# Score products of levels 2 to 6 by head, each head on its own half of TensorE's rows

## The reference

```python
def _attn_ref(q, k, v, f_logit):            # (4, 8, 768, 48)
    f = 1.0 / (1.0 + np.exp(-f_logit))
    state = np.zeros((B, H, D, D))
    for t in range(S):
        state = f[:, :, t, :, None] * state + np.einsum('bhd,bhe->bhde', k[:, :, t], v[:, :, t])
        y[:, :, t] = np.einsum('bhd,bhde->bhe', q[:, :, t], state)

def _moe_ref(x, w_in, w_out):               # (3072, 384) x (384, 2048) x (2048, 384)
    h = x @ w_in
    return (h * (1.0 / (1.0 + np.exp(-1.702 * h)))) @ w_out

def _moe2_ref(x, domain_probs, w1, w2):     # 4 experts, 384 -> 1024 -> 384
    p = domain_probs / (domain_probs.sum(-1, keepdims=True) + 1e-09)
    for e in range(E):
        out += p[:, e:e + 1] * (np.maximum(x @ w1[e], 0.0) @ w2[e])
```

## Time and profile before

| | |
|---|---|
| time, median of 3 runs | 1414.91 us (1414.72 to 1416.94) |
| profiled execution | 1414.12 us, of it the span 1412.4 us |
| granted clock of TensorE | 0.999 of full speed |
| PE busy | 1386.7 us, 98% of the span |
| DVE, POOL, ACT busy | 913.5, 629.6, 568.4 us |
| line 1580 | 960 pairs: 120 from half 0, 840 from halves 1 to 7 |
| share of line 1580 in the chain that ended last | 7% |

### The profile page before, as it was taken

How to read it: one execution, slowest core, us unless ns; L and a number is a source line. 1 busy time by engine, 2 the same in 40 slices (tenths; PEclk the granted TensorE clock), 3 DMA queues, 4 the chain that set the end, 5 groups by cost and what they waited for, 6 DMA issues and landing times.

```text
span 1412.4 us, 20981 instructions
## 1 busy us (share of the span) xinstructions
PE 1386.7 (98%) x8092; PEld 1311.8 (93%) x8092; DVE 913.5 (65%) x1376; ACT 568.4 (40%) x975; POOL 629.6 (45%) x719
## 2 busy tenths in 40 slices
PE   6899999999999999999999999999999999999999
PEld 5799999999999999999999999999999999999998
DVE  7785747566665656356566666666666666666666
ACT  5563534344444445245333233332333333433331
POOL 8686645556564747265512122211212454344430
PEclk9999999999999999999999999999999999999999
DMA  9535243332425160121011010101011112222111
GB/s 156 121 84 83 60 60 79 47 92 36 103 26 113 16 114 13 41 90 51 23 34 35 12 34 23 34 12 34 12 34 56 35 34 67 91 68 67 46 57 45
DMA packets 239796, 79.00 MB, mean 56 GB/s; under 512 B 188752, under 2 KB 238160, under 8 KB 239696
## 3 DMA queue, kind: packets, MB, share of 16 engines
q1 hardware_dynamic: 239696, 77.66, 23.9%
HBM read 67.83 MB, written 9.78 MB: 55 GB/s over the span
## 4 chain that ended last, share of the span: by engine, by line
PE 94%; POOL 2%; issue 1%; DVE 1%; ACT 1%; SPq 1%; DMA 0%; POOLq 0%; DVEq 0%; ACTq 0%
PE bank L1766 9%; PE bank L1764 9%; PE bank L1765 9%; PE bank L1700 9%; PE bank L1701 9%; PE bank L1699 9%; PE bank L1580 7%; PE bank L1672 5%; PE bank L1673 5%; PE bank L1674 5%; PE bank L1506 4%; PE bank L1508 4%; PE bank L1507 4%; PE bank L1612 3%; PE bank L1620 1%; PE bank L1629 1%
## 5 line engine op out<-in xcount | busy, mean ns | idle before, releaser
L1460 DVE SCALAR_TENSOR_TENSOR acc<-bank,p_n,acc 128x384 f32<-128x384 f32 x384 | 235.0, 612 | 68.0 <-PE bank L1766 62.9
L788 POOL TENSOR_TENSOR g_l<-sig,g_h 128x384 fp32r<-128x384 f32 x128 | 163.8, 1280 | 228.6 <-ACT g_h L1027 228.6
L1766 PE MATMUL bank<-w_h,h_l 128*128 128x384 f32 x768 | 257.3, 335 | 0.0
L1764 PE MATMUL bank<-w_h,h_h 128*128 128x384 f32 x768 | 257.2, 335 | 0.0
L1765 PE MATMUL bank<-w_l,h_h 128*128 128x384 f32 x768 | 257.0, 335 | 0.0
L1444 DVE TENSOR_TENSOR bank<-bank,x_copy 128x512 f32<-128x512 f32 x192 | 124.5, 694 | 166.0 <-ACT x_copy L1124 102.4
L1701 PE MATMUL bank<-xs,we_l 128*128 128x512 f32 x528 | 206.5, 391 | 0.0
L1700 PE MATMUL bank<-xs,we_h 128*128 128x512 f32 x528 | 206.4, 391 | 0.0
L1699 PE MATMUL bank<-xs,we_h 128*128 128x512 f32 x528 | 205.5, 389 | 0.7 <-issue 0.7
L839 POOL TENSOR_TENSOR we_l<-we_raw,we_h 128x384 fp32r<-128x384 f32 x96 | 97.2, 1037 | 213.4 <-ACT we_h L1092 213.4
L1356 DVE TENSOR_TENSOR sig<-bank,sig 128x384 f32<-128x384 f32 x128 | 71.0, 555 | 162.8 <-ACT sig L1020 161.4
(11 more groups left out here) (145 smaller groups left out, 2567.1 us busy)
## 6 DMA issues: line engine op xcount, KB each, us to landing
we_raw<-in_moe_w SPq DMA_DIRECT2D x32, 384.0 KB, 4.0
w_raw<-in_moe_w SPq DMA_DIRECT2D x32, 384.0 KB, 3.3
v_sb<-in_v SPq DMA_DIRECT2D x24, 192.0 KB, 3.5
x_dram<-work SPq DMA_DIRECT2D x8, 576.0 KB, 3.1
x_raw<-x_dram SPq DMA_DIRECT2D x12, 384.0 KB, 4.0
f_raw<-in_f_logit SPq DMA_DIRECT2D x56, 72.0 KB, 2.1
q_raw<-in_q SPq DMA_DIRECT2D x56, 72.0 KB, 2.1
k_raw<-in_k SPq DMA_DIRECT2D x56, 72.0 KB, 2.0
```

Source lines behind the costliest of these rows:

```text
L788: pool.tensor_tensor(g_l[:, j % RING, :], sig[:, j % 2, :], g_h[:, j % RING, :].bitcast(F32), ALU.subtract).then_inc(gl_ready, 1)
L1460: dve.scalar_tensor_tensor(acc[:, pr * TT + i, :], y_bank[y % 3][:, 0:DM], p_n[:, col:col + 1], acc[:, pr * TT + i, :], ALU.mult, ALU.add) ...
L1764: pe.matmul(dst, hh, wh, start=f == 0, stop=False)
L1766: last = pe.matmul(dst, hl, wh, start=False, stop=f == 1)
```

## The change

From half 1 on, `level_by_heads` takes the place of the loop over chunks. Each score product is done per head: weights are the head's 48 rows of `k_T`, 128 columns of them, and the streamed operand is the head's 64 columns of `q_split`. `tile_position=(0, 0)` for even and `(64, 0)` for odd heads places them on the upper or the lower 64 rows of the array. A level has 24 products of 64 columns instead of 12 of 128, so 48 recorded pairs instead of 24. For level 6 only the first 64 key positions are loaded (`rows`), since only they are wanted.

The banks no longer hold one chunk each. The bank `odd` holds the odd heads of chunks 0 and 1, `even` their even heads, and `last` both heads of chunk 2 in turn; upper and lower rows never write the same bank at a time, and before the odd heads of chunk 2 go into `last` TensorE waits for `upper_ready`. The readers get at their scores through `scores_of`, with as many elements as before. `unit_ready` is raised after products 16, 23 and 24 of the level's 24; before, it was raised after 4, 8 and 12 of 12. The level waits at its start for the banks `last` and `odd` and after eight products for `even`; before, each chunk waited for its own.

```diff
+    def scores_of(i, n):
+        if n == 0 or i == CH - 1:
+            return scores_T[:, i, :, :]
+        by_two = scores_T[:, 0:2, :, :].rearrange("p c (r j) x -> p (c r) j x", j=2)
+        return by_two[:, :, 1 - i, :]
...
-                    done = act.activation(scores_T[lo:lo + m, i, :, lo + m:lo + 2 * m],
+                    done = act.activation(scores_of(i, n)[lo:lo + m, :, lo + m:lo + 2 * m],
...
-                        dst = scores_T[:, i, :, :].rearrange("p h (b a m) -> p h b a m", a=2, m=m)[:, :, :, 1, :]
+                        dst = scores_of(i, n).rearrange("p h (b a m) -> p h b a m", a=2, m=m)[:, :, :, 1, :]
...
+            def level_by_heads(L, n):
+                odd, even, last = (level_unit[L] + i for i in range(CH))
+                def head(u, at, ch, r, j):
+                    x, lo = r * CH + ch, GAP * j
+                    rows = HALF_CH if L == LEVELS - 1 else P
+                    return pe.matmul(ring[u % 3][0:rows, at * HALF_CH:(at + 1) * HALF_CH],
+                                     k_T[lo:lo + D, x * P:x * P + rows], q_split[lo:lo + D, x, j, :],
+                                     start=True, stop=True, tile_position=(lo, 0))
+                bank_free(last, n)
+                bank_free(odd, n)
+                pe.wait_ge(split_ready, (n * (LEVELS - FIRST) + L - FIRST + 1) * 2 * CH)
+                pe.wait_ge(kg_ready, (n * LEVELS + L) * CH)
+                for r in range(PAIRS):
+                    upper = head(last, 2 * r, 2, r, 0)
+                    if r == PAIRS - 1:
+                        upper.then_inc(upper_ready, 1)
+                    head(odd, r, 0, r, 1)
+                bank_free(even, n)
+                for r in range(PAIRS):
+                    head(even, r, 0, r, 0)
+                    lower = head(odd, PAIRS + r, 1, r, 1)
+                lower.then_inc(unit_ready, 1)
+                for r in range(PAIRS):
+                    upper = head(even, PAIRS + r, 1, r, 0)
+                    if r == PAIRS - 1:
+                        upper.then_inc(unit_ready, 1)
+                    if r == 0:
+                        pe.wait_ge(upper_ready, (n - 1) * (LEVELS - FIRST) + L - FIRST + 1)
+                    lower = head(last, 2 * r + 1, 2, r, 1)
+                lower.then_inc(unit_ready, 1)
...
-                    if L < FIRST and not fine(n):
+                    if not fine(n):
+                        if L >= FIRST:
+                            level_by_heads(L, n)
                         return
```

More of the change, by code:

```diff
@@ L383, in moe_of_attention_kernel @@
         w_hi_ready, w_lo = sem("w_hi_ready"), {"pool": sem("w_lo_by_pool"), "dve": sem("w_lo_by_dve")}
-        unit_ready = sem("unit_ready")
+        unit_ready, upper_ready = sem("unit_ready"), sem("upper_ready")
         read_by = {"act": sem("act_read"), "dve": sem("dve_read")}
@@ L1569, in step @@
                         bank_free(u, n)
[L1570 to L1577, removed]
+                        pe.wait_ge(split_ready, (L - FIRST) * 2 * CH + 2 * (ch + 1))
+                        pe.wait_ge(kg_ready, (L - 1) * CH + ch + 1)
                         for r in range(PAIRS):
```

## The result

The changed kernel takes 1422.13 us (median of four runs, 1420.99 to 1423.69) against 1414.82 (1413.97 to 1416.94): 7.3 us slower, ratio 1.005 with an interval of 1.0033 to 1.0068. It is inside the forecast range of 1405 to 1502, on the slow side, and 4.6 us above the predicted 1417.5. The profiled execution took 1420.99 us, its span is 1419.3.

A forecast was written before the change was run, and what follows sets the result against it. TensorE was taken to bound the kernel. Terms 0 - 9.4 + 6.0 + 3.9 + 2.1 = +2.6 us on the profiled 1414.1 gave 1416.7, and 0.8 for the median made 1417.5 us; range 1405 to 1502.

The forecast's parts named there:

- the case: Loads of upper and lower rows run side by side: 1417.5 us, from 1405 to 1434, chance 48%.
- its signs: Profile after: levels 2 to 5 at 2.8 to 3.0 us, level 6 at 1.6 to 1.8, TensorE idle before level 6.
- loads in series: Rival: the array takes one weight load at a time, +81 us, 1496 us, chance 33%.
- (c): Entering and leaving a level changes the array's shape: 0.17 us a level, +6.0 us, range 0 to +12.
- (b): Level 6 loads only 64 weight columns, so it takes half the time: -1.34 us a level, -9.4 us.
- (d): At each level the lower half starts and ends one step later: 0.11 us a level, +3.9 us, or 0.
- (a): Levels 2 to 5: doubled loads run side by side in both halves, 0 us; one after the other, +75 us.
- (e): Later `unit_ready` delays ScalarE's squares at level 5, so TensorE waits 0.3 us before level 6: +2.1 us.
- Each half twice as quick: Rival: shorter loads make a level 1.34 us, -35 us in all, 1380 us, chance 13%.

The follow-up runs named there:

- level 6 alone: Only level 6 goes by heads, all other levels as in the kernel before: 1414.02 us against 1416.69, ratio 0.998.
- the kernel with the bands late: Kernel before with level 6 by heads and GpSimd's last small cross products and VectorE's sum moved behind tile 7's low part: 1436.86 us, ratio 1.0146.
- the second attempt's control: Kernel before, whole height, with GpSimd's low part of tile 7 ahead of its level 6 fade and k_rows transposes one slot later: 1419.82 us, ratio 1.0045.

## Why the prediction was right, and where it was off

The sum was +2.6 us and the outcome +7.3; the case was the forecast one, and its signs came: 2.83 and 1.61 us for the levels in the chain, 0.27 us at an entry, and an idle time ahead of level 6. That the time fell into the range says little by itself, since the range had to hold the loads in series too. That the sum is off by no more than 4.7 us is in part luck: (c), the gain of (b) and the missed wait were too favourable by 3.9, 1.2 and 1.1 us, (d) was too dear by 2.2.

**(a), loads side by side: right.** 48 pairs in the time of 24, and 4.90 us when each half's products stand together. This was the 75 us of the question, and the trace of before could not decide it; the argument that nothing shown as shared is asked for twice held, and the condition that it named, consecutive products on opposite halves, turned out to be needed. The Trainium skill (TensorEngine Tiling (Array Packing), Key Properties) says that different tiles load and multiply in parallel; the trace agrees where the halves alternate, 0.059 us a pair.

**(b), level 6: right, slightly too large.** 1.40 us from first to last matmul instead of 2.57, -1.17 a level where -1.34 stood: the step in each half is 0.059, not 0.056, and the first pair of the level is slower. -8.2 instead of -9.4 us.

**(c), the changes of shape: the mis-sized term.** I put 0.17 us a level, half of the 0 to 0.34 from the rows. The entry costs 0.10 and the exit 0.20, 0.30 together at levels 2 to 5 and 0.24 at level 6: +9.9 instead of +6.0 us, near the upper end. The same section of that page says that a change of the tiling mode drains TensorE. The trace agrees: the next load isn't started early, and each edge costs time. By that rule I had +8.6 us for the sum, and that is nearer to the 7.3 than my own value. The reason not to trust it, that no row of before showed such a change, was a reason for a wide range and none for the middle.

**(d), the second half starts a step late: wrong mechanism.** At levels 2 to 5 both halves start and end together, 0.007 us apart. A level is 0.06 us longer from its first to its last start, at its first pair, not 0.11: +1.7 us instead of +3.9.

**(e), the wait for ScalarE: right in place and size**, 0.31 us a half for 0.3 predicted, +2.2 for +2.1, and shown by level 5 whole against by heads. The size is in part luck: the squares start 0.91 us later in the level and not 0.7, but level 5 itself lasts longer, which gives ScalarE most of the difference back. Missed: GpSimd. I wrote that the time of its unit stays, which holds for the time within a level. But in the kernel before the low part of tile 7 was ready less than 0.1 us ahead of its use in `layer_out` (258.10 and 258.16), at the end of a chain over VectorE and GpSimd, and anything that delays these relative to TensorE, or makes TensorE earlier, ends in a wait there. In the changed kernel that is 0.16 us a half, +1.1; with level 6 alone it took 4.7 of 6.5 us.

The rivals: loads in series did not come, and would have with the same products in another order. Each half twice as quick is refuted at levels 2 to 5, where a half's step is 0.112 as ever; it is the load that bounds, and it goes by columns (0.112, 0.085 and 0.059 us a step at 128, 96 and 64) and not by rows. The chance of 61% for slower was right.

## What to carry to other kernels

Before two products are placed side by side, ask which of load and streaming sets the step: halving the streamed columns gains nothing while each product needs as many weight columns as before, and the gain comes only where both shrink. Count the edges: an excursion into another shape of the array costs 0.24 to 0.34 us here, so it needs at least that much work saved inside. Put products that are to overlap next to each other in the program: TensorE looked only some three pairs ahead. And a gain on the bounding engine stops at the next engine's margin: look for work that arrives within 0.1 us of its use, and for what stands in order ahead of it, before summing gains over halves.

## What the runs showed of the hardware that was not expected

- Weights of 128 rows by 64 columns, and not only half the rows, made TensorE pay as for a change of shape: 0.27 us at the entry instead of 0.17.
- With twelve products on the upper rows followed by twelve on the lower, pairs of the two halves overlapped only around the change, seven of the 48; TensorE began with the lower ones three pairs early.
- With half of the rows at work at a time, TensorE had matmuls in flight for 99.7 of 100 us, and its clock was granted at 1.2 GHz in stretches of that time, mean 0.86. With both halves at work in turn it stayed at 2.4 GHz through the same levels. What sets this apart was not studied further.
- Behind idle times of about 2 us in each half (the kernel with the bands late) the clock was granted at 1.2 GHz for 3 to 7 us, though TensorE was busy again when it fell. Behind the 0.7 us in each half of the second attempt's control it stayed at 2.4 GHz.
- At levels 2 to 5 two pairs on opposite halves start within a hundredth of a microsecond of each other, 48 in 2.83 us.
